# A second buffer for split weight sums, moved loads and side work in the down-projections, and another order at the end of attention

## What is computed

```
scores = q @ k.T / 8 + (cum[:, None] - cum[None, :])     # cum = cumsum(log(clip(f))), causal mask
x = softmax(scores) @ v                                  # -> 2304 tokens x 512
xn = x / sqrt(mean(x*x) + 1e-6) * rms_g
y = (silu(xn @ w_gate) * (xn @ w_val)) @ w_out           # 512 -> 1536 -> 512
h = y @ w_in                                             # 512 -> 2048
out = silu(h) @ w_out2                                   # 2048 -> 512
```

## Time and profile before

| | us |
|---|---|
| median of 3 runs | 1037.66 |
| lowest and highest of them | 1034.42 and 1037.98 |
| the profiled execution | 1032.13 |
| its span, first to last instruction | 1030.3 |
| TensorE busy in the span | 989.9 (96%) |
| mean granted TensorE clock | 0.992 |

### The profile page before, as it was taken

The page is one execution under the profiler, slowest core; times in us unless marked ns, Lnnn a source line. Parts: engine busy times, 40 slices in busy tenths (PEclk is TensorE's granted clock), DMA queues, the critical chain, the costliest instruction groups (busy, mean ns, idle before and its releaser), DMA issues.

```text
span 1030.3 us, 16304 instructions
## 1 busy us (share of the span) xinstructions
PE 989.9 (96%) x5904; PEld 899.0 (87%) x5904; DVE 646.4 (63%) x1264; ACT 451.7 (44%) x968; POOL 314.0 (30%) x248
## 2 busy tenths in 40 slices
PE   5999999898899879999999999999999999999998
PEld 4777777697799879999999999998989889898996
DVE  5777778477647839778878189751756327562451
ACT  4776687534335314434324235252543326243350
POOL 2665543321311146433524235112030211302112
PEclk9999999999899989999999999999999999999999
DMA  7466545256713656657857757545243544534312
GB/s 240 152 222 186 158 144 172 68 193 248 273 63 150 248 225 235 245 213 279 285 219 255 262 213 249 192 174 194 111 185 134 188 180 163 190 108 182 154 31 92
DMA packets 58591, 192.58 MB, mean 187 GB/s; under 512 B 8272, under 2 KB 19024, under 8 KB 52368
## 3 DMA queue, kind: packets, MB, share of 16 engines
q1 hardware_dynamic: 58512, 191.54, 51.9%
HBM read 150.02 MB, written 41.49 MB: 186 GB/s over the span
## 4 chain that ended last, share of the span: by engine, by line
PE 79%; DVE 7%; DMA 5%; ACT 3%; issue 3%; POOL 2%; SPq 1%; DVEq 0%; ACTq 0%; POOLq 0%
PE banks L1668 15%; PE banks L1670 14%; PE banks L1669 14%; PE banks L1801 6%; PE banks L1800 6%; PE banks L1799 6%; PE banks L1614 4%; PE banks L1582 4%; PE banks L1553 4%; DMA kept<-ws 3%; PE banks L1556 1%; DMA stage_d<-w 1%; DVE scratch L1402 1%; POOL wd L751 1%; DVE ws L1245 1%
## 5 line engine op out<-in xcount | busy, mean ns | idle before, releaser
L1668 PE MATMUL banks<-xb,wu 128*128 128x384 f32 x864 | 289.2, 335 | 5.5 <-DVE x_sb L1170 2.9
L1670 PE MATMUL banks<-xb,wu 128*128 128x384 f32 x864 | 288.7, 334 | 0.0
L1669 PE MATMUL banks<-xb,wu 128*128 128x384 f32 x864 | 288.7, 334 | 0.0
L751 POOL TENSOR_TENSOR wd<-stage_d,wd 128x512 fp32r<-128x512 f32 x84 | 120.0, 1436 | 490.4 <-ACT wd L934 490.4
L1668 PEld LDWEIGHTS banks<-xb,wu 128*128 128x128 f32 x864 | 162.2, 188 | 6.7 <-DVE x_sb L1170 3.0
L1669 PEld LDWEIGHTS banks<-xb,wu 128*128 128x128 f32 x864 | 162.2, 188 | 0.2
L1670 PEld LDWEIGHTS banks<-xb,wu 128*128 128x128 f32 x864 | 162.2, 188 | 0.0
L993 ACT ACTIVATE scratch<-scratch 128x384 f32<-128x384 f32 x144 | 75.4, 523 | 112.9 <-DVE scratch L1360 51.1
L1002 ACT ACTIVATE hid_main<-scratch 128x384 fp32r<-128x384 f32 x144 | 72.2, 517 | 117.1 <-DVE scratch L1402 117.1
L1668 PE MATMUL banks<-hid_main,wd 128*128 128x384 f32 x288 | 100.6, 349 | 19.6 <-POOL wd L751 19.6
L1409 DVE TENSOR_TENSOR hid_main<-scratch,hid_main 128x384 fp32r<-128x384 f32 x144 | 88.3, 627 | 40.6 <-ACT hid_main L1002 36.3
(11 more groups left out here) (163 smaller groups left out, 1698.8 us busy)
## 6 DMA issues: line engine op xcount, KB each, us to landing
wu<-kept SPq DMA_DIRECT2D x48, 1792.0 KB, 10.8
stage_d<-w SPq DMA_DIRECT2D x84, 256.0 KB, 2.8
kept<-ws SPq DMA_DIRECT2D x20, 1024.0 KB, 5.3
qk_raw<-qk_t SPq DMA_DIRECT2D x16, 576.0 KB, 3.5
cum_b<-cum_dram SPq DMA_DIRECT2D x32, 288.0 KB, 5.4
kept<-wu SPq DMA_DIRECT2D x12, 768.0 KB, 4.3
kept<-ws SPq DMA_DIRECT2D x8, 768.0 KB, 5.3
v_sb<-v_p SPq DMA_DIRECT2D x16, 320.0 KB, 4.6
```

Of the source, the lines that this page charges most:

```text
L751: nc.gpsimd.tensor_tensor(wd[:, d % 2, 1, :], stage_d[:, d % 2, :], f32(wd[:, d % 2, 0, :]), ALU.subtract).then_inc(wd_split, 1)
L1668: nc.tensor.matmul(dst, w_hi_part, m_hi, start=start, stop=False)
L1669: nc.tensor.matmul(dst, w_hi_part, m_lo, start=False, stop=False)
L1670: return nc.tensor.matmul(dst, w_lo_part, m_hi, start=False, stop=stop)
```

## The change

It has four parts. (1) The sums of odd units q = 1, 3 to 11 get a buffer of their own, which lies in blocks 4 to 6 of `xb[:, 0]` (T3, T1 and T4 of the x blocks, unused until span 1), with its own semaphore; `xt_high` of span 1 therefore waits until all six stores from it have landed. (2) At the end of attention the high and low parts of B21, B12 and B22 and the normalisations before them are moved to earlier places, and TensorE's wait for the end of attention, which stood before everything else of cycle 0, is split into one before C12 and one before C22. (3) SyncE's order: `load_down(1, 4)` and `(1, 5)` before `load_unit(12)`; in final plain cycles the first sums are stored before the two loads and `load_up` goes before the last sums; the next unit of the second layer is loaded after the raw part is stored, not after the sums. (4) In half 3 and 5 the job of the down-projection stands behind its last `w_down` on ScalarE and GpSimd, as it did in half 1.

```diff
-        ws_out = sem("ws_out")
+        ws_out = [sem(f"ws_out{b}") for b in range(2)]
+        def ws_of(q):
+            if q < UNITS1 and q % 2 == 1:
+                return xb[:, 0, 4:7].rearrange("p a c t -> p (a c t)")[:, 0:2 * SUMS].rearrange("p (b n) -> p b n", b=2)
+            return ws
+        def ws_sem(q):
+            return ws_out[q % 2 if q < UNITS1 else 0]
         def ws_outs(q, part):
-            return q + 1 if q < UNITS1 else UNITS1 + 2 * (q - UNITS1) + (1 if part == "raw" else 2)
+            return q // 2 + 1 if q < UNITS1 else UNITS1 // 2 + 2 * (q - UNITS1) + (1 if part == "raw" else 2)
...
@@ SyncE, job(slot) @@
                     if part == "raw":
                         keep_raw(q)
+                        if q + 1 < UNITS1 + UNITS2:
+                            load_unit(q + 1)
                     else:
                         keep_sums(q)
-                        if q + 1 < UNITS1 + UNITS2:
-                            load_unit(q + 1)
@@ SyncE, the halves @@
+                    sums = SUMS_IN_CYCLE.get(n, ())
+                    for q in sums[:1]:
+                        keep_and_load(q)
                     if n == final:
                         load_down(g, 2)
                         load_down(g, 3)
-                    for q in SUMS_IN_CYCLE.get(n, ()):
-                        keep_and_load(q)
                     if PLAIN <= n + 1 < NCYC and n != CYCLES_OF[g][0]:
                         load_up(n + 1)
+                    for q in sums[1:]:
+                        keep_and_load(q)
...
                 else:
+                    for c in range(4, CHUNKS_OF[g]):
+                        load_down(g, c)
                     if g == 1:
                         load_unit(UNITS1)
-                    for c in range(4, CHUNKS_OF[g]):
-                        load_down(g, c)
@@ GpSimd @@
                 row_sums(p)
+                if p == NPAIRS - 1:
+                    xb_lo(0, "B12")
                 spread_factors(p)
-            xb_lo(0, "B12")
             xb_lo(0, "B22")
...
-                elif g > 1:
+                elif g % 2 == 0:
                     job(("down", g))
...
-                elif g == 1:
+                elif g % 2 == 1:
                     job(("down", g))
@@ ScalarE (the two edits of job(("down", g)) also here) @@
             def xt_high(x, name):
...
+                if x == 1:
+                    act.wait_ge(ws_out[1], 16 * (UNITS1 // 2))
...
             def w_sums(q):
                 act.wait_ge(s_made, 4 * q + 4)
-                wait(act, ws_out, 16 * (ws_outs(q, "sums") - 1))
+                wait(act, ws_sem(q), 16 * (ws_outs(q, "sums") - 1))
...
-                nc.scalar.activation(ws[:, 0, :], stage_of(q), ACT.Copy).then_inc(sums_hi, 1)
+                nc.scalar.activation(ws_of(q)[:, 0, :], stage_of(q), ACT.Copy).then_inc(sums_hi, 1)
@@ ScalarE, the pairs @@
                 if p == NPAIRS - 1:
                     xb_high(0, "B11")
+                    xb_high(0, "B21")
...
                 if p == NPAIRS - 1:
-                    xb_high(0, "B21")
+                    xb_high(0, "B12")
                 if here:
                     take_out(p, "t0")
+                if p == NPAIRS - 1:
+                    xb_high(0, "B22")
...
-                if p == NPAIRS:
-                    xb_high(0, "B12")
-                    xb_high(0, "B22")
@@ VectorE: normalise_x of span 0 moved @@
# (0, 3, 0) at p = 15: from behind shift(p, 8) to behind invert(p - 1)
# (0, 0, 1) at p = 15: from the end of the turn to behind shift(p, 8)
# (0, 2, 1), (0, 3, 1) at p = 16: from the end to in front of take_out(p - 1, "t1")
@@ TensorE @@
-            pe.wait_ge(x_done, 2 * NPAIRS)
-            pe.wait_ge(out_act, copies(len(TURN) - 1, True))
-            pe.wait_ge(out_dve, copies(len(TURN) - 1, False))
...
                         for c in PLAIN_ORDER:
+                            if n == 0 and c == 3:
+                                pe.wait_ge(out_act, copies(len(TURN) - 1, True))
+                                pe.wait_ge(out_dve, copies(len(TURN) - 1, False))
+                            if n == 0 and c == 1:
+                                pe.wait_ge(x_done, 2 * NPAIRS)
```

More of the change, by code:

```diff
@@ L542, in keep_raw @@
                 else:
-                    sp.dma_start(dst, f32(ws[:, :, 0:RAW])).then_inc(ws_out, 16)
+                    sp.dma_start(dst, f32(ws[:, :, 0:RAW])).then_inc(ws_out[0], 16)
             def keep_sums(q):
                 sp.wait_ge(sums_split, q + 1)
-                sp.dma_start(kept[q:q + 1, :, :, RAW:].rearrange("a p b n -> (a p) b n"), f32(ws[:, :, :])).then_inc(ws_out, 16)
+                sp.dma_start(kept[q:q + 1, :, :, RAW:].rearrange("a p b n -> (a p) b n"), f32(ws_of(q)[:, :, :])).then_inc(ws_sem(q), 16)
             def load_up(n):
@@ L553, in load_up @@
                     q = unit_of(n, u)
-                    sp.wait_ge(ws_out, 16 * ws_outs(q, "sums"))
+                    sp.wait_ge(ws_sem(q), 16 * ws_outs(q, "sums"))
                     if first_layer(n):
@@ L904, in w_raw @@
                     act.wait_ge(unit_in[q % 2], 48 * (len(range(q % 2, UNITS1, STAGES1)) + (q - UNITS1) // 2 + 1))
-                    act.wait_ge(ws_out, 16 * (ws_outs(q, "raw") - 1))
+                    act.wait_ge(ws_out[0], 16 * (ws_outs(q, "raw") - 1))
                     if (q, "raw") == AFTER_MEAN:
@@ L1085, in _ @@
                     w_down(g, 3)
-                if g > 1:
+                if g % 2 == 0:
                     job(("down", g))
@@ L1092, in _ @@
                     w_down(g, c)
-                if g == 1:
+                if g % 2 == 1:
                     job(("down", g))
@@ L1244, in w_sums @@
                 dve.wait_ge(sums_hi, q + 1)
-                nc.vector.tensor_tensor(ws[:, 1, :], stage_of(q), f32(ws[:, 0, :]), ALU.subtract).then_inc(sums_split, 1)
+                nc.vector.tensor_tensor(ws_of(q)[:, 1, :], stage_of(q), f32(ws_of(q)[:, 0, :]), ALU.subtract).then_inc(sums_split, 1)
             def s_sums(q):
@@ L1277, in _ @@
                     normalise_x(0, 2, 0)
+                if p == NPAIRS:
+                    normalise_x(0, 2, 1)
+                    normalise_x(0, 3, 1)
                 if p > 0:
@@ L1290, in _ @@
                     qk_round(p + 1)
+                if p == GUESS_PAIR + 4:
+                    normalise_x(0, 3, 0)
                 if here:
@@ L1313, in _ @@
                     normalise_x(0, 1, 0)
-                if p == GUESS_PAIR + 4:
-                    normalise_x(0, 3, 0)
+                if p == NPAIRS - 1:
+                    normalise_x(0, 0, 1)
                 if following:
@@ L1325, in _ @@
                 if p == NPAIRS - 1:
-                    normalise_x(0, 0, 1)
                     normalise_x(0, 1, 1)
-                if p == NPAIRS:
-                    normalise_x(0, 2, 1)
-                    normalise_x(0, 3, 1)
             def split_squares(span):
                 dve.wait_ge(sq_step, 2 * (2 * DC - 1) + span * (2 * DC - 1))
-                dve.wait_ge(ws_out, 16 * ws_outs(*(SUMS_IN_DOWN[1], "sums") if span == 1 else BEFORE_MEAN))
+                dve.wait_ge(ws_out[0], 16 * ws_outs(*(SUMS_IN_DOWN[0], "sums") if span == 1 else BEFORE_MEAN))
                 nc.vector.tensor_copy(norm_split(span, 0), norm_tmp(span, 0)).then_inc(ss_hi_done, 1)
```

## The result

The changed kernel took 1004.57 us (median of 4 runs, 1003.72 to 1005.26) against 1036.04 of the kernel before beside it (1032.63 to 1037.98): a ratio of 0.971, 95% interval 0.9684 to 0.9737. The profiled execution went from 1032.13 to 1003.89 us and its span from 1030.3 to 1002.1: 28.2 less, where 24.9 were forecast. Two of the four runs on the other chip (1009.62 and 1010.59) lie some 5 us above all the others; the experiments come to that.

A forecast was written before the change was run, and what follows sets the result against it. TensorE was busy 989.9 of 1030.3 us, so only idle time and slow clock could be won: 12.1 (through the first down-projection) + 9.4 (second) + 3.4 (fourth, sixth) = 24.9; 1037.66 - 24.9 = 1012.8 us, range 1005 to 1022.

The forecast's parts named there:

- The walk through both lists: Plain cycles before the first down-projection: ScalarE's and VectorE's lists followed in order; three store waits of 8.8 give 6.5 us.
- (a): First down-projection, chunk 0: it needs the banks of cycle 2's last outputs and loses about 1.3 us.
- (b): First down-projection, chunk 2: high copy 12.0 us after the first, piece ready 256.2 instead of 254.5, loses 1.7 us.
- (c): First down-projection, chunk 3: its copy is now bound by VectorE's sums, loses 0.9 us.
- (d): First down-projection, chunk 4: GpSimd has 3.5 us of squares before it, loses 0.9 us.
- (e): First down-projection, chunk 5: last piece lands near 271 after 6.3 MB of requests, loses 2.6 us (bounds 0 and 4).
- rival E: Cycles 9, 12 and 15: load_up's pair behind a unit makes it slower, 1046 us if each costs 11; chance 0.02.
- rival A: Second down-projection: T2's new store wait replaces the load's, 8.6 of the 24.9 us lost, 1021.4; chance 0.12.
- B: First down-projection: transfers bound it, gaps over 3 us and clock down, some 5 us more lost, 1018; chance 0.12.
- C: Second buffer brings nothing since VectorE's sums bound the list; the other parts win 17.4 us, 1020; chance 0.09.
- F: Stores still hold the copies, load order doesn't matter; only attention, fourth and sixth win, 8 us, 1029.6; chance 0.03.
- D: VectorE's and ScalarE's lists run better than walked; first down-projection loses 2 instead of 7.4 us, 1007; chance 0.06.

The follow-up runs named there:

- u_unit: The changed kernel with the second layer's units loaded after the stores of the sums again: 1008.91 us, ratio 0.973.
- u_job: The changed kernel with the jobs of halves 3 and 5 put back before piece 4 on ScalarE and GpSimd: 1012.92 us.
- a_order: The kernel before with SyncE's order alone, without the earlier load of the second layer's units: 1021.72 us, ratio 0.9885.
- a_buffer: The kernel before with the second buffer for the sums alone, including xt_high's wait on its stores: 1022.02 us, ratio 0.989.
- x_piece3: The changed kernel with piece 3's high copy of the second down-projection ahead of xt_high T2 and T3 on ScalarE: 1002.65 us, ratio 0.968.
- p_buffer: x_piece3 with one buffer for the sums, the second taken out: 1011.56 us, ratio 0.9778.
- x_best: x_piece3 with, in the first down-projection, pieces 2 and 3 earlier on ScalarE and piece 4's load ahead of two raw stores: 1006.33 us, ratio 0.9716.
- x_best2: x_piece3 with x_best's ScalarE order, GpSimd's squares behind piece 4, loads of pieces 4 and 5 ahead of the stores: 1002.68 us, ratio 0.9697.

## Why the prediction was right, point by point

- **The parts and their sum.** The forecast was 1012.8, range 1005 to 1022; measured were 1004.6 and 1007.3, that is 28 to 31 us less instead of 24.9. The first of these lies 0.4 below the range and both below the 1009 to 1016 that had most of the chance. Of the 8.2 us between 1012.8 and 1004.6, 3.3 are the sum (1007.2 forecast for the profiled execution, 1003.89 measured). The other 4.9 come from the step to the timed median: it lay 5.5 above the profiled execution in the kernel before, the forecast kept that distance, and in the changed kernel it is 0.7. Alone the parts gave 5.5, 11.4 and 11.8, and the jobs 3.4 from the stages: 32 together in timed medians, and 4.0 + 8.5 + 10.4 + 3.4 = 26.3 by the profiled spans, of which the whole change took 28.2. So they add up to within a few us.
- **End of attention.** 4.65 forecast, 6.19 - 1.13 = 5.06 measured. The 0.2 for the copy ahead of pair 15's take-outs didn't show.
- **To the first down-projection.** 5.25 forecast (9.9 - 4.65), 5.16 measured. That this is right to 0.1 us is TensorE's doing: with the weights ready in time the stretch is 22 products at 2.08, whenever exactly the list gets there. The walk through both lists has its own measure, the high copy of piece 0. It ran at 239.03; 241.4 less the 1.1 of the start and the 0.4 of attention is 239.9. So the walk was 0.9 too cautious, 7.4 us gained in this stretch where it had 6.5, and the three waits together (8.8) would have been 1.4 too much. ScalarE's sums wait for VectorE now, 1.7 before those of units 2 and 4, as said, and no store.

```profile
236.99 1.06 ACT L932 ACTIVATE ws<-scratch 128x1024 fp32r<-128x1024 f32 x1 [1.69 <-DVE scratch L1271]
```

- **First down-projection.** 2.2 forecast, 5.43 measured; it lost 4.5 us against the 25.0 of its matmuls, not 7.4. By the starts of the chunks, step (a) is 0.6 where 1.3 was forecast, (b) 1.35 where 1.7, (c) 1.0 where 0.9 and (d) 1.3 where 0.9. The causes of (b) and (c) are those named. Chunk 4's wait (d) was to come from GpSimd's squares, but ScalarE got the piece only at 262.22, after 5.14 us of waiting for its transfer, and the squares were over by 262.54, so the transfer ended this wait, with the squares 0.4 us away from it:

```profile
262.22 0.63 ACT L949 ACTIVATE wd<-stage_d 128x512 fp32r<-128x512 f32 x1 [5.14 <-DMA stage_d<-w]
...
266.68 0.63 ACT L949 ACTIVATE wd<-stage_d 128x512 fp32r<-128x512 f32 x1 [2.31 <-DMA stage_d<-w]
```

The mis-sized term is (e). I let piece 5 land near 271, 18.3 us after the requests began at 252.7, for 6.3 MB at 350 GB/s. The requests began at 250.43 and ScalarE had the piece at 266.68, 16.2 us later. It did wait for it, 2.31 us, but its chunk didn't, so 2.6 became 0, the lower bound given. That was close: GpSimd was through with the piece at 268.67 and the chunk began at 268.74. The error is in the bytes and not in the rate: a unit is loaded in three transfers of 256, 128 and 128 KB, 512 KB in all, and the prediction counts 1024 KB for it. The requests up to piece 5 are 5.2 MB, and the trace has them at a mean of 323 GB/s, less than the 350 supposed. With 5.2 MB at 350 the prediction's own sum would have had the piece 3 us earlier, in time for its chunk. The rows are the loads of the two units (KB each, median us to landing) and the stretch (columns as in the earlier trace rows):

```profile
stage_u<-w SPq DMA_DIRECT2D x2, 256.0 KB, 3.8
stage_u<-w SPq DMA_DIRECT2D x4, 128.0 KB, 3.6
```

```profile
250.43:266.68 16.25, 13.35 (x74) 12.39 (x74) 12.75 (x12) 4.41 (x6) 8.95 (x5) 1.00 0.87 323
```

The same 1024 KB stands in the paragraph on the second down-projection's waits, in that on the moved loads and in rival E (4.7 MB); there it changed no conclusion.
- **Second down-projection.** 9.4 forecast, 8.05 and 8.88 measured in the two shorter outcomes (27.63 and 26.80), 3.6 in the long one (32.04 and 32.10, in u_unit and u_job). The load's wait went as said. The added wait of T2 was priced at 0.2 with an upper bound of 3. "I am wrong if T2 waits for a store" was a sign named beforehand, and it came, as did a wait over 2 us in this stretch. This step of the mechanism was wrong, at a price that the rest of the sum covers. The row shows it:

```profile
334.29 1.58 ACT L906 ACTIVATE xb<-scratch 128x768 fp32r<-128x768 f32 x2 [3.63 <-DMA kept<-xb]
```

The store was issued at 329.22 and took 5.1, as supposed (4 to 5.5), while VectorE had T2 ready at 333.1: 1.2 late. What I had not seen is what follows. In the kernel before, piece 3's low part ran in the middle of VectorE's two-input subtractions as well, but it began 0.32 us ahead of the next of them (352.61 and 352.93), took 1.53 us, and VectorE's took 2.02. The 1.2 us carry it to 0.05 us before a subtraction, and there it takes 1.27, 2.12 or 4.72. That is rival A's place with a smaller price: T2 did wait for its store, though that stood behind no other transfer. a_order, which has no such wait, has a gap of 0.99 here, and a_buffer, which has it, one of 2.37; with the copy ahead of T2 (x_piece3) there is none, and the 0.97 of before is gone too. The three prices fit a port that VectorE and GpSimd share; no run takes VectorE's subtractions away to test it. The Trainium skill ("SBUF — State Buffer", section "SBUF: two separate sides") has the one that comes later fully blocked for an instruction. 1.27 beside VectorE's 2.03 agrees with that, and so does 2.12, which is one of VectorE's more; 4.72 does not: there GpSimd stood behind four, back to back. I had weighed this rule for a microsecond in the first down-projection and not here.
- **Fourth and sixth.** 3.4 forecast, 1.75 + 1.70 measured. The moved loads cost nothing, as said (u_unit).
- **Rivals.** B (transfers bound the first down-projection) came only at chunk 4, with 1.03 us and no gap over 3, and C (VectorE bounds the list) didn't come; a_buffer and p_buffer exclude C. F is excluded by the parts alone. D supposed a first down-projection that loses 2; it lost 4.5, between D and the forecast. E: no cycle waited for `wu`.

What stays open: which of the three outcomes the second down-projection takes. In all of them the instructions of ScalarE, GpSimd and VectorE around it begin at the same distances to 0.05 us, and nothing that was looked at in the profiles before them tells them apart.

## What to carry to other kernels

When a wait for a store or load is taken out of an engine that runs in order, walk that engine's list and its partner's with measured durations: it came to within 0.9 us here (6.5 for 7.4), where the sum of the waits (8.8) would have been 1.4 too high. Take the bytes of a transfer from the profile before you price a queue: a size twice too large made a wait of 2.6 us that didn't exist. Ask of each new wait not only what it delays but into what neighbour's work it pushes the next instruction: 1.2 us of delay cost a gap of 1.5 or 2.4 us, or one of 5 with half clock, and putting the one urgent copy ahead of the wait removed it all. A transfer of megabytes belongs where nobody asks for a small one within its landing time; moving one pair of loads by 12 us was worth 9 to 11 us.

## What was not expected of the hardware

The granted clock doesn't follow from the length of one gap. After 2.90 us of waiting at 203.88 the kernel before kept 2.4 GHz; the kernel with the buffer alone waited the same 2.90 at 203.84 and got a mean of 0.66 in the next 5 us, and a_order, with 2.90 at 203.74, kept 1.00 over the same 5 us. x_best fell to 1.2 GHz after a gap of 1.80, x_best2 after one of 2.80, and the changed kernel stayed at full clock after 2.37. The stretches of a_buffer and of x_best2:

```profile
204.00:209.00 5.00, 5.00 (x21) 5.00 (x22) 1.96 (x1) 3.93 (x5) 3.77 (x3) 0.66 0.02 3
```

```profile
269.00:275.00 6.00, 5.81 (x24) 5.81 (x25) 1.68 (x3) 1.76 (x4) 3.39 (x3) 0.72 0.81 263
```

And one instruction of GpSimd, the low part of piece 3, took 1.27, 2.12 and 4.72 us (the last in two kernels) beside VectorE's run, with the same neighbours at the same distances.
